# Attention and two dense layers on one core: VectorE's reciprocal of three row sums is issued behind the low parts of the tile instead of in front of them

## The reference

```python
# attention, 2 x 8 heads, 768 rows, head size 64, 6 hash bits
mask = q_bucket[:, :, :, None] == k_bucket[:, :, None, :]
scores = scale * np.matmul(q, k.transpose(0, 1, 3, 2))
scores = np.where(mask, scores, -1000000000.0)
scores = scores - np.max(scores, axis=-1, keepdims=True)
attn = np.exp(scores)
attn = attn / (np.sum(attn, axis=-1, keepdims=True) + 1e-09)
out = np.matmul(attn, v).astype(np.float32)
# then x (1536 x 512) goes through two dense layers, 512 -> 2048 -> 512
g = np.where(pos, h, np.where(neg, 0.0, (h + beta) ** 2 / (4.0 * beta)))   # first
g = h - np.tanh(h)                                                        # second
```

## Time and profile before

| what | value |
|---|---|
| median of 3 runs | 797.55 us (797.17 to 797.69) |
| profiled execution | 796.39 us, its span 794.4 us |
| TensorE busy | 765.7 us (96%) |
| VectorE busy | 422.4 us (53%) |
| ScalarE busy | 355.0 us (45%) |
| Pool busy | 326.3 us (41%) |

### The profile page before, as it was taken

One profiled execution on the slowest core, in us unless ns is written; L12 is line 12 of the kernel. 1 busy time (PEld: TensorE's weight loads), 2 busy tenths in 40 slices (PEclk: granted clock), 3 DMA queues, 4 the chain that ended last, 5 costly groups with the idle time before them and its releaser, 6 DMA issues.

```text
span 794.4 us, 11750 instructions
## 1 busy us (share of the span) xinstructions
PE 765.7 (96%) x3712; PEld 637.0 (80%) x3712; DVE 422.4 (53%) x757; ACT 355.0 (45%) x701; POOL 326.3 (41%) x267
## 2 busy tenths in 40 slices
PE   4999999999999999999999999999999999999997
PEld 2788888888888788878887888778888888888885
DVE  2999999999996665343334455541213222222222
ACT  2888889889885333333334323331212212222121
POOL 4789889899899993000000267760000000000000
PEclk8999999999999999999999999999999999999999
DMA  5533423433132332000000022210001000010001
GB/s 193 179 103 112 152 78 116 145 104 104 61 98 80 133 110 78 0 1 1 0 1 0 26 86 99 98 61 1 1 0 42 11 0 0 0 53 0 0 0 53
DMA packets 17864, 47.25 MB, mean 59 GB/s; under 512 B 2288, under 2 KB 4464, under 8 KB 17840
## 3 DMA queue, kind: packets, MB, share of 16 engines
q1 hardware_dynamic: 17840, 46.94, 18.4%
HBM read 38.87 MB, written 3.15 MB: 53 GB/s over the span
## 4 chain that ended last, share of the span: by engine, by line
PE 80%; POOL 5%; issue 5%; DVE 4%; ACT 3%; DMA 2%; SPq 1%; DVEq 0%; POOLq 0%; ACTq 0%
PE ps L489 33%; PE ps L564 30%; PE ps L466 5%; PE ps L480 5%; PE ps L452 2%; PE ps L455 2%; PE ps L423 2%; POOL probs L346 2%; POOL k_b L331 1%; ACT probs L610 1%; DMA k_raw<-kk 1%; DVE g_raw L805 1%; ACT g_hi L692 1%; DVE row_den L735 1%; POOL q_b L303 1%
## 5 line engine op out<-in xcount | busy, mean ns | idle before, releaser
L489 PE MATMUL ps<-x_hi,w 128*128 (+1 forms) x768 | 255.0, 396 | 0.0
L813 DVE TENSOR_TENSOR g_lo<-g_raw,g_hi 128x512 fp32r<-128x512 f32 x96 | 72.4, 754 | 268.5 <-ACT g_hi L692 268.5
L692 ACT ACTIVATE g_hi<-g_raw 128x512 fp32r<-128x512 f32 x96 | 60.8, 633 | 294.9 <-PE ps L564 266.3
L489 PEld LDWEIGHTS ps<-x_hi,w 128*128 128x128 f32 x768 | 144.4, 188 | 33.9
L489 PE MATMUL ps<-x_lo,w 128*128 (+1 forms) x384 | 152.1, 396 | 0.0
L564 PE MATMUL ps<-g_hi,w 128*128 128x512 f32 x384 | 125.6, 391 | 3.1 <-DVE g_lo L813 3.1
L564 PE MATMUL ps<-w,g_hi 128*128 128x512 f32 x384 | 118.6, 390 | 0.0
L303 POOL TENSOR_SCALAR w<-stage 128x1024 fp32r<-128x1024 f32 x32 | 38.1, 1191 | 165.4 <-PE ps L564 163.5
L743 DVE TENSOR_TENSOR p_lo<-ps,p_hi 128x384 fp32r<-128x384 f32 x192 | 97.8, 551 | 9.6 <-ACT p_hi L620 7.7
L346 POOL TENSOR_SCALAR probs<-probs,row_inv 128x768 f32<-128x768 f32 x96 | 86.9, 909 | 23.5 <-DVE row_inv L737 23.5
L620 ACT ACTIVATE p_hi<-ps 128x384 fp32r<-128x384 f32 x192 | 84.7, 489 | 24.3 <-PE ps L466 22.7
(11 more groups left out here) (48 smaller groups left out, 900.8 us busy)
## 6 DMA issues: line engine op xcount, KB each, us to landing
stage<-weights SPq DMA_DIRECT2D x32, 512.0 KB, 3.3
qk_raw<-qk SPq DMA_DIRECT2D x16, 384.0 KB, 3.5
q_raw<-qq SPq DMA_DIRECT2D x16, 384.0 KB, 3.2
k_raw<-kk SPq DMA_DIRECT2D x16, 384.0 KB, 3.8
q_a<-q_b SPq DMA_DIRECT2D x16, 192.0 KB
v_raw<-v SPq DMA_DIRECT2D x16, 192.0 KB, 2.4
out<-stage SPq DMA_DIRECT2D x12, 256.0 KB, 2.3
q_b<-bits SPq DMA_DIRECT2D x16, 54.0 KB
```

What stands on the lines that cost most here:

```text
L489: last = nc.tensor.matmul(ps[:, f % H_BANKS, :], w[:, f, wp, k * P:(k + 1) * P], xs[:, :, k, bass.ds(t * TOK, TOK)], start=(k == 0 and wp ...
L692: nc.scalar.activation(g_hi[:, slot, :], g_raw[:, slot, :], ACT.Copy).then_inc(g_hi_ready, 1)
L813: nc.vector.tensor_tensor(g_lo[:, slot, :], g_raw[:, slot, :], g_hi[:, slot, :].bitcast(F32), ALU.subtract).then_inc(g_split, 1)
```

## The change

In VectorE's turn, `invert` is called after `parts_lo` and no longer before it. Both keep their conditions, so that they are issued in the same turns as before. The wait of `invert` for the exponentials goes with it. No other engine's order changes.

```diff
@@ -771,12 +771,12 @@
                     old = trailing(p, n, FOLD_LAG)
                     if n % HT == HT - 1 and old and not (drain and n >= FOLD_LAG):
                         fold(old[0], old[1] // HT)
+                    old = trailing(p, n, TRANSPOSE_LAG)
+                    if old and not (drain and n >= TRANSPOSE_LAG):
+                        parts_lo(*old)
                     old = trailing(p, n, HT)
                     if n % HT == 0 and old and not (drain and n >= HT):
                         invert(old[0], old[1] // HT)
-                    old = trailing(p, n, TRANSPOSE_LAG)
-                    if old and not (drain and n >= TRANSPOSE_LAG):
-                        parts_lo(*old)
                     if not drain and n in BITS_AFTER and not last:
                         threshold(p + 1, BITS_AFTER.index(n))
```

## The result

The changed kernel takes 808.88 us (median of 4 runs, 808.52 to 808.92), the kernel before 797.52 us on the same chip; the ratio is 1.0143, with an interval of 1.0128 to 1.0158. It is slower by 11.4 us, and 808.1 had been forecast. The profiled execution took 808.91 us, its span is 807.0 us, 12.6 more than before.

The account below looks back on a forecast made before the run. The bound was taken to be the once-per-pair loop through Pool's scalings, which wait for row_inv. 8.8 + 1.0 + 0.8 = 10.6 us on the 797.55 us median gave 808.1 us, 8-in-10 range 803.5 to 810.5.

Parts of the forecast that it names:

- The place: Attention stage only: the dependency loop through Pool closes once per head pair; its loss reaches the end one for one.
- Sites 6 and 9: VectorE's turns 6 and 9, where row_den and row_inv stand: Pool's scaling starts 1.43 and 1.46 us later.
- site 3: Where row_den and row_inv stand in VectorE's turn 3: Pool idles some 0.4 us more, where TensorE has 0.8 to spare.
- Site 0: Where row_den and row_inv stand in VectorE's turn 0: Pool's subtraction catches row_den, Pool scales 1.46 us later.
- the list: VectorE's turn 0: three arrivals, copied bits included, meet within 0.1 us; each can only push row_den into Pool's subtraction.
- From site 0 to TensorE: Pool busy from turn 0's scaling to TensorE's transposes: loop 1.46 us longer; TensorE's 0.41 us p_lo wait goes, given back later.
- The sum: Whole attention stage: 6 x 1.46 = 8.8, plus 1.0 at the first such place, plus 0.8 in the last pair: 10.6 us.
- To site 0 of pair 1: First turn 0 with the small pair: Pool's longer earlier wait, 0.84 against 0.44, absorbs 0.4 of the shift; 1.0 us left.
- The last pair: Pool's split of w holds row_den, the clamp comes 1.6 us later, TensorE's 0.76 us wait absorbs half: 0.8 us.
- `row_den` slips in first: VectorE's turn 0: row_den precedes Pool's subtraction, costing 1.02 a pair, 7.7 us in all, 805.3; chance 0.3.
- VectorE is the bound: VectorE's stretch without pauses: blocked row_den leaves p_lo's way, 1.37 x 6 = 8.2 us less, 789.3; chance 0.07.
- waits only change hands: Around the pair: Pool's delays vanish in its existing waits, 0.2 us a pair either way, 796.5 to 799; chance 0.07.

Follow-up runs that it names:

- the variant with the reciprocal: The changed kernel with row_den computed by a reciprocal and not by an addition, scaling by the row sum itself: 804.64 us, ratio 1.0096.

## Why the prediction was right, step by step

**The place.** Right. The dense part kept its length within 0.03 us, Pool's work is the same, and the loop through Pool's queue got longer, once a pair. One sign that the prediction named did not come: Pool's waits grew to 36.5 us and not to over 40. Its own waits by site (3.1, 0.8, 0.4 and 0.4 us, against 1.7, 0.75 and 0.44 before) add some 1.8 us a pair, 11 us in six, which makes about 35, so its own terms did not give the "over 40".

**Sites 6 and 9.** Right. Pool's wait at site 6 is 2.66 us (1.68 + 1.43 = 3.1 less 0.4 which Pool lost just before at site 3), at site 9 it is 0.77, and at site 9 the small pair stands in VectorE's stretch without pauses.

**Site 0.** Right in its result: `row_den` is caught, and site 9 to site 0 is again 7.30 us on Pool, which the sum asked for. One arrival was not on the list. VectorE's fold at 162.38 waits for Pool's split of x, late by the same shift, and so `p_lo` stands at 164.65 right behind the clamp. The listed one would have been enough: `p_hi` was started at 164.05, 0.52 later is 164.57, and 0.94 after that 165.51, still behind Pool's 165.41, by 0.10 us. So the tie was as close as the forecast had it, and that it fell this way owes something to luck; the fold's wait made the margin 0.18. The scores of turn 0 started at 162.01, 2.64 us after the issue of the copy at 159.37; 2.41 had been taken from the earlier trace rows. TensorE idled 0.13 us before them, and the trace does not say for what, so whether the copied bits held them back stays open.

**From site 0 to TensorE.** Right in the main: TensorE waits 0.92 and 0.41 us for a scaled tile, where before it waited once, at the 166.24 of the earlier trace rows. The larger wait is one scaled tile earlier than forecast. TensorE's wait for `p_lo` was to go; it is gone in turn 1, but 0.24 us of waiting for `p_lo` come back one turn later, at 168.16. `row_den` at site 3 is held by Pool's own scaling for 0.37 us more than it takes, and Pool idles 0.44, as forecast, at no cost.

**The sum.** A pair: 1.46 forecast, 1.43 measured, six times 8.6 (Pool's scalings at site 0, from pair 1 to pair 7: 42.04 to 217.30 before, 44.30 to 228.15 after). The two ends are the terms that were sized too low. To site 0 of pair 1: 1.0 forecast, 1.84 measured (27.52 - 25.68). The forecast took the steady shift and subtracted Pool's longer wait; but Pool was already idle at that site, so `p_lo` and its wait for `p_hi` delay it in full. In the variant that moves site 0 alone Pool's scaling there starts 27.00 us after the first scores (43.39 - 16.39), 1.3 later. With sites 6 and 9 alone moved it is 0.8 later; the sum of both would be 2.1, so here too the sites do not add up. The last pair: 0.8 forecast, 1.8 measured (of 12.63 us at TensorE's last wait, 10.85 were there at 228.15). The clamp came 1.84 us later and not 1.6, TensorE's wait for Pool's scaling of 0.76 us went, as forecast, and at the transposes behind it (238.92 before, 250.89 now) the shift is 11.97 us, 1.1 in this pair. What the forecast left out comes next: TensorE's wait for `p_lo`, 0.50 us before, is 1.06 in the changed kernel.

```profile
243.05 0.92 PE L466 MATMUL ps<-ident,probs 128*128 128x128 f32 x6 [0.50 <-DVE p_lo L743]
```

```profile
255.68 0.92 PE L466 MATMUL ps<-ident,probs 128*128 128x128 f32 x6 [1.06 <-DVE p_lo L743]
```

That `p_lo` stands behind a fold on VectorE, and the fold behind Pool's split of x, which itself follows a scaling for which Pool waited 1.24 us at site 9. It is the same arrival that was missing from the list at site 0:

```profile
254.52 0.55 DVE L754 TENSOR_TENSOR x_pair<-ps,low 64x384 f32<-64x384 f32 x1 [0.32 <-POOL x_lo L351]
254.99 1.00 DVE L743 TENSOR_TENSOR p_lo<-ps,p_hi 128x384 fp32r<-128x384 f32 x2
```

The remaining 0.4 us of the profile's 12.6 are the first loads, which came 0.42 us later in this execution (first scores at 16.78, not 16.36). So the profile's 12.6 is 8.6 + 1.8 + 1.8 + 0.4, the median's 11.4 a little less than that without the loads (12.2): the two profiled executions are 0.8 us further apart than the medians are, which stays open. That the forecast total is within 0.8 us of the measured one (10.6 and 11.4) is in part luck: by the traces its terms were 1.6 us short (10.6 and 12.2).

**The rivals.** That `row_den` slips in first is excluded for the changed kernel. Its price is confirmed by the variant with the reciprocal, in which nothing slips in but nothing is held: 804.64, where 805.3 was worked out. That VectorE is the bound, or that waits only change hands, is excluded by the pair of 30.64 us.

## What to carry to other kernels

An instruction that takes 0.2 us can set the length of a loop of 30: ask who waits for it, and what that engine does next, before it is moved behind something longer. A place inside another wait is free; a place behind the instruction that had waited is not, and delays whoever waits by that instruction's whole length. Delays of several sites do not add up: each is first taken out of the idle time of the waiting engine at the next site. So work out the loop once around, and the first and last turns by themselves.

## What the runs showed of the hardware

A `TENSOR_SCALAR` of 128 x 3 numbers from SBUF to SBUF on VectorE waits for the end of the Pool instruction that is running, be it a scaling, a rounding or a subtraction. It took 0.16 us with Pool idle and 1.82 us at the most, and each one held ended 0.02 to 0.03 us after Pool's instruction. A `RECIPROCAL` of the same shape in the same place took 0.16 to 0.17 us at all 32 sites, one of them 0.16 us into a subtraction of Pool. The Trainium skill, "VectorE: DVE Perf Modes", section "The perf-mode tier table (the rule you actually need)", gives `tensor_scalar` on fp32 in SBUF twice the base rate. With the lock that was cited ahead, the runs agree for the form that is held. That a reciprocal is not held is what the runs show, and no run shows in which mode either form ran. The `TENSOR_SCALAR` was worth 4.4 us of the kernel before (797.31 to 792.94); by the steps of Pool above, 0.44 us a pair of that was the hold and 0.19 the instruction's own time.
